# Gram products ahead of the merge, keys in four loads, one head per Gram matmul

## The reference, cut to what matters

```python
# r, k, v, w, a, b: [4 batches, 8 heads, 768 tokens, 40]
for t in range(S):
    y[:, :, t] = einsum('bhd,bhde->bhe', r_t, state)
    Sa = einsum('bhde,bhe->bhd', state, a_t)
    state = state * w_t[:, :, None, :] - einsum('bhd,bhe->bhde', Sa, b_t) \
            + einsum('bhd,bhe->bhde', v_t, k_t)
# then on y: x @ w_in, relu, a convolution of 3 taps over the tokens, a gate, @ w_out,
# and per batch an FFT over tokens and width, a normalization, and two more matmuls
```

## Time and profile before

| | us |
|---|---|
| median of 3 runs (1068.22 to 1072.94) | 1071.59 |
| the profiled execution's own time | 1070.56 |
| its span | 1068.7 |
| PE busy in it | 874.5 |
| DVE busy in it | 627.3 |
| ACT busy in it | 455.8 |
| POOL busy in it | 246.4 |

### The profile page before, as it was taken

One profiled execution on the slowest core, in us unless ns is written; L12 is line 12 of the kernel. 1 busy time (PEld: TensorE's weight loads), 2 busy tenths in 40 slices (PEclk: granted clock), 3 DMA queues, 4 the chain that ended last, 5 costly groups with the idle time before them and its releaser, 6 DMA issues.

```text
span 1068.7 us, 26585 instructions
## 1 busy us (share of the span) xinstructions
PE 874.5 (82%) x11476; PEld 829.9 (78%) x11476; DVE 627.3 (59%) x1109; ACT 455.8 (43%) x791; POOL 246.4 (23%) x236
## 2 busy tenths in 40 slices
PE   1658878878789699796686799887998779988798
PEld 1657777777778688795685799877998769987698
DVE  3684974965966957904596514765137652377522
ACT  2437356365365274273663313643136421264211
POOL 4326336245345353324232200000000000000000
PEclk9859989989979889889797899988999979998899
DMA  9501351451351351161331101001010010100001
GB/s 296 198 21 42 127 164 42 127 164 42 126 164 47 122 165 42 22 194 40 100 99 37 45 1 37 1 1 45 1 37 1 1 34 11 38 1 1 1 1 37
DMA packets 46245, 71.46 MB, mean 67 GB/s; under 512 B 27105, under 2 KB 37986, under 8 KB 42210
## 3 DMA queue, kind: packets, MB, share of 16 engines
q1 hardware_dynamic: 46130, 69.77, 20.4%
HBM read 61.89 MB, written 7.86 MB: 65 GB/s over the span
## 4 chain that ended last, share of the span: by engine, by line
PE 38%; DVE 11%; ACT 3%; issue 1%; DMA 0%; POOL 0%; SPq 0%; DVEq 0%; POOLq 0%; ACTq 0%
PE psum L1164 16%; PE psum L1172 15%; PE psum L1213 3%; PE psum L1232 2%; DVE gs L1035 2%; DVE cv L1081 1%; DVE cv L1079 1%; ACT cv L962 1%; PE psum L1155 1%; DVE stats L1122 1%; DVE tok L1050 1%; DVE gf L1089 1%; ACT hp L956 1%; DMA tok<-y_scratch 0%; DVE res L1117 0%
## 5 line engine op out<-in xcount | busy, mean ns | idle before, releaser
L1164 PE MATMUL psum<-xs,w 128*128 128x384 f32 x1152 | 216.9, 342 | 21.2 <-DVE xs L1071 12.2
L1172 PE MATMUL psum<-w,gs 128*128 128x320 f32 x1296 | 207.9, 316 | 18.6 <-DVE gs L1035 18.5
L1164 PEld LDWEIGHTS psum<-xs,w 128*128 128x128 f32 x1152 | 203.2, 191 | 23.6 <-DVE xs L1071 12.3
L1172 PEld LDWEIGHTS psum<-w,gs 128*128 128x128 f32 x1296 | 199.6, 193 | 22.4 <-DVE gs L1035 17.5
L1143 DVE SCALAR_TENSOR_TENSOR gs<-psum,gs 128x384 fp32r<-128x384 f32 x80 | 44.7, 558 | 151.6 <-ACT gs L1009 151.6
L1009 ACT ACTIVATE gs<-psum 128x384 fp32r<-128x384 f32 x80 | 39.3, 491 | 157.3 <-PE psum L1164 157.3
L472 DVE TENSOR_TENSOR inv<-inv,outer 128x31 f32<-128x31 f32 (+15 forms) x186 | 98.5, 529 | 6.4
L379 POOL TENSOR_TENSOR score<-score,mask 128x512 f32<-128x512 f32 x48 | 65.6, 1388 | 127.6 <-ACT score L594 127.5
L470 DVE TENSOR_TENSOR outer<-low,inv 128x31 f32<-128x31 f32 (+15 forms) x186 | 80.5, 433 | 4.5
L455 DVE TENSOR_TENSOR gram_k<-bank,mask 128x512 f32<-128x512 f32 x24 | 16.6, 692 | 110.8 <-PE bank L640 110.8
L900 POOL MEMSET xs<- 128x217 f32 x8 | 2.0, 278 | 285.4 <-ACT hp L956 285.4
(11 more groups left out here) (120 smaller groups left out, 1613.1 us busy)
## 6 DMA issues: line engine op xcount, KB each, us to landing
kb<-in_kb SPq DMA_DIRECT2D x6, 2048.0 KB, 8.5
rt<-in_rt SPq DMA_DIRECT2D x12, 1024.0 KB, 5.9
w_in<-in_w SPq DMA_DIRECT2D x6, 1040.5 KB, 9.9
at<-in_a SPq DMA_DIRECT2D x6, 1024.0 KB, 5.5
zt<-in_vt SPq DMA_DIRECT2D x12, 512.0 KB, 7.7
v_tok<-in_v SPq DMA_DIRECT2D x6, 640.0 KB, 7.7
y_scratch<-y_t SPq DMA_DIRECT2D x48, 80.0 KB
out<-res SPq DMA_DIRECT2D x24, 160.0 KB, 1.9
```

The lines of the kernel that those rows point to most:

```text
L1164: last = mm(ps[6 + half][:, 0:HALF], a[:, 128 * f:128 * f + 128], x[:, HALF * half:HALF * (half + 1)], start=(i == 0), stop=(i == len(ever ...
L1172: last = mm(ps[t][:, 0:DM], gs[:, f % 2, x, 128 * t:128 * t + 128], w[:, y, f, :], start=(f == 0 and i == 0), stop=(f == count - 1 and i = ...
```

## The change

`attention_jobs` gets a new order, `vector_order` goes, and `prep` is cut into `scan` (one for each b), `at`, `decays`, `eye` and `ends`. The copies `odd` and `blank` and the second half of the tile `at` go. A Gram matmul takes one head, with 64 rows of the array; the heads of one bank are those of eight pairs, the two row halves alternating with the two column halves. The minus-signed products are kept in two tiles (`gram_b`, `gram_m`), and `inv_1`, `merged` move to a tile of their own. The diagonal copies become a job `diag`, behind `mt`, and swap the heads of a pair for one chunk. `kb` is loaded in four pieces.

```diff
+    def grams(g, halves=range(2)):
+        return [("gram", g, kind, 2 * half + flip) for half in halves for kind in (0, 1) for flip in range(2)] if g < STEPS else []
...
+    def merge(g, beside):
+        order = each("mj", g, 0, 2) + beside + each("mt", g, 0, 2) + one("diag", g)
+        return order + [("pu", g, half, b) for b in batches for half in range(2)]
+
+    SUBS = (0, 10, 11, 17, 28, Q - 1)
+
+    order = each("scan", 0) + one("at", 0) + one("decays", 0) + each("keys", 0) + one("ends", 0)
+    order += interleave(grams(0), each("scan", 1)) + each("ta", 0) + one("eye", 0) + one("split", 0)
+    early = each("tb", 0, 1) + each("tb", 0, 0) + each("akv", 0) + one("at", 1) + one("decays", 1) + each("keys", 1)
+    order += interleave(early, subs(0, 0, 26)) + one("ends", 1) + interleave(grams(1), subs(0, 26, Q - 1))
+    order += one("unsplit", 0) + one("eye", 1) + merge(0, []) + one("split", 1) + subs(1, 0, SUBS[1])
     for g in range(STEPS):
         if g + 1 < STEPS:
-            order += interleave(grams(g + 1), state(g, 0, ("sat", "sa")))
-            beside = interleave(state(g, 0, ("st", "xn", "y", "xt")) + state(g, 1, ("sat", "sa", "st", "xn")),
-                                tokens(g + 1)[:-NB])
-            order += interleave(beside, chain(g + 1)[:-1]) + state(g, 1, ("y",)) + chain(g + 1)[-1:] + prep(g + 2)
-            order += merge(g + 1)[:2] + tokens(g + 1)[-NB:] + merge(g + 1)[2:] + spread(g + 1) + state(g, 1, ("xt",))
+            order += one("decays", g + 1) if g else []
+            first = interleave(each("sat", g, 0, 2) + each("sa", g, 0), each("ta", g + 1) + each("tb", g + 1, 1))
+            first += each("st", g, 0)
+            order += interleave(first, each("scan", g + 2) + subs(g + 1, SUBS[1], SUBS[2]))
+            second = each("xn", g, 0) + zipped(each("y", g, 0), each("tb", g + 1, 0)) + each("xt", g, 0, 2)
+            order += interleave(second, subs(g + 1, SUBS[2], SUBS[3])) + one("at", g + 2)
+            keys = each("keys", g + 2)
+            third = interleave(each("sat", g, 1, 2) + each("sa", g, 1), each("akv", g + 1)) + keys[0:2]
+            third += each("st", g, 1) + keys[2:4] + each("xn", g, 1)
+            order += interleave(third, subs(g + 1, SUBS[3], SUBS[4])) + one("ends", g + 2)
+            order += interleave(each("y", g, 1), subs(g + 1, SUBS[4], SUBS[5])) + one("unsplit", g + 1) + one("eye", g + 2)
+            last = grams(g + 2, (1,))
+            order += grams(g + 2, (0,)) + last[:2] + merge(g + 1, last[2:] + each("xt", g, 1, 2))
+            order += one("split", g + 2) + subs(g + 2, 0, SUBS[1])
...
@@ SyncE
-            if stage == "gram" and (c, b) == (0, NB - 1) and more:
+            if stage == "scan" and b == NB - 1 and more:
+                load_w(g + 1)
+            if stage == "ta" and b == NB - 1 and more:
                 load_a(g + 1)
             if stage == "akv" and b == NB - 1 and more:
-                load_w(g + 1)
                 load_v(g + 1)
-            if stage == "tb" and (c, b) == (1, NB - 1) and more:
-                load_kb(g + 1)
+            if stage == "tb" and c == 0 and more:
+                load_kb(g + 1, b)
...
@@ ScalarE
-                nc.scalar.mul(gram_b[0:2 * Q, heads, :], grams[0:2 * Q], -1.0)
-                nc.scalar.mul(gram_b[2 * Q:4 * Q, heads, 0:Q], grams[2 * Q:4 * Q, :, Q:C], -1.0).then_inc(drained[bank], 1)
+                nc.scalar.mul(gram_b[:, slots_b, :], grams[:, :, 0:Q], -1.0)
...
+                nc.scalar.mul(gram_m[:, g % 2, slots_b, :], grams[0:2 * Q, :, Q:C], -1.0).then_inc(drained[bank], 1)
...
@@ TensorE
-                for i, n in enumerate(pairs):
...
+                for i in range(NH):
+                    n = b // 2 * NH + i
+                    for q in range(1 if c == 0 else 2):
                         for cc in range(2):
+                            k = (b + cc) % 2
+                            r = slice(C * k, C * k + C)
+                            if c == 0:
+                                last = mm(out[C * cc:C * cc + C, i, :], kb[r, n, cc, 0, :],
+                                          at_quarters[r, n, :, cc, :], start=True, stop=True)
+                            else:
                                 p = Q * (2 * q + cc)
+                                last = mm(out[p:p + Q, i, 0:C - Q * q], kb[r, n, cc, 1, Q * q:Q * q + Q],
+                                          at_quarters[r, n, q:2, cc, :], start=True, stop=True)
```

More of the change, by code:

```diff
@@ L63, in attention_jobs, with each, one, subs @@
     batches = range(NB)
-    def prep(g):
-        return [("prep", g, 0, 0)] + [("keys", g, 0, b) for b in batches] if g < STEPS else []
-    def grams(g):
-        jobs = [("odd", g, 0, 0)] + [(stage, g, 0, b) for b in batches for stage in ("ta", "blank")]
-        return jobs + [("gram", g, kind, b) for kind in (1, 0) for b in batches]
-    def chain(g):
-        return [("split", g, 0, 0)] + [("sub", g, 0, i) for i in range(Q - 1)] + [("unsplit", g, 0, 0)]
-    def tokens(g):
-        jobs = [(stage, g, 0, b) for stage in ("akv",) for b in batches]
-        return jobs + [("tb", g, c, b) for c in range(2) for b in batches]
-    def merge(g):
-        return [("mj", g, 0, 0), ("mj", g, 0, 1), ("mt", g, 0, 0), ("mt", g, 0, 1)]
-    def spread(g):
-        return [("pu", g, half, b) for b in batches for half in range(2)]
-    def state(g, c, stages):
-        return [(stage, g, c, b) for stage in stages
-                for b in range(2 if stage in ("sat", "xt") else NB)]
+    def each(stage, g, c=0, n=NB):
+        return [(stage, g, c, b) for b in range(n)] if g < STEPS else []
+    def one(stage, g):
+        return [(stage, g, 0, 0)] if g < STEPS else []
+    def grams(g, halves=range(2)):
+        return [("gram", g, kind, 2 * half + flip) for half in halves for kind in (0, 1) for flip in range(2)] if g < STEPS else []
+    def subs(g, lo, hi):
+        return [("sub", g, 0, i) for i in range(lo, hi)] if g < STEPS else []
     def interleave(a, b):
@@ L115, in attention_jobs @@
-    return order
-def vector_order(order):
-    out, held = [], []
-    for job in order:
-        if job[0] == "y" and job[2] == 1 and job[1] + 1 < STEPS:
-            held.append(job)
-        else:
-            out.append(job)
-        if job[0] == "unsplit":
-            out += held
-            held = []
-    return out
-NOT_PSUM = ("prep", "table", "keys", "odd", "blank", "split", "sub", "unsplit")
+            order += one("decays", g + 1) if g else []
+            first = interleave(each("sat", g, 0, 2) + each("sa", g, 0), each("ta", g + 1) + each("tb", g + 1, 1))
@@ new lines, in attention_jobs @@
+            order += interleave(third, subs(g + 1, SUBS[3], SUBS[4])) + one("ends", g + 2)
[3 more added lines that the diff above has]
+            order += one("split", g + 2) + subs(g + 2, 0, SUBS[1])
+        else:
+            order += [(stage, g, 0, b) for stage in ("sat", "sa", "st") for b in range(2 if stage == "sat" else NB)]
+            rest = each("xn", g, 0) + each("y", g, 0) + each("xt", g, 0, 2)
+            rest += each("sat", g, 1, 2) + each("sa", g, 1) + each("st", g, 1)
+            order += interleave(rest, [("table", g, 0, i) for i in range(FIRST_PIECES)])
+            order += each("y", g, 1)
@@ L135, in first_tables @@
+    return order
+NOT_PSUM = ("scan", "at", "decays", "keys", "ends", "eye", "table", "split", "sub", "unsplit", "diag")
 def first_tables(nc, ctx, dram):
@@ L208, in attention @@
     s_a = sem("s_a")
-    s_kb = sem("s_kb")
+    s_kb = [sem(f"s_kb{i}") for i in range(NB)]
     s_rt = [sem(f"s_rt{c}") for c in range(2)]
@@ L302, in _ @@
         sp.dma_start(ident[:, :], dram["ident"]).then_inc(s_const, 16)
-        load_kb(0)
+        for b in range(NB):
+            load_kb(0, b)
         sp.dma_start(mask[:, :], dram["mask"]).then_inc(s_const, 16)
@@ L415, in _ @@
         dve.wait_ge(s_slots, 3)
-        for job in vector_order(order):
+        for job in order:
             stage, g, c, b = job
-            if stage == "prep":
+            if stage == "scan":
                 dve.wait_ge(s_w, 16 * (g + 1))
```

150 lines of the change are left out of this document (71 added, 79 removed).

## The result

The changed kernel takes 1114.97 us (median, 1106.96 to 1120.8), the kernel before 1072.26 us beside it on the same chip (1068.22 to 1073.4): a ratio of 1.04, interval 1.0328 to 1.0472. It is slower by 42.7 us, and the forecast of 1078 us and its range up to 1098 us both miss it. The profiled execution has a span of 1105.2 us against 1068.7 us: 36.5 us more. It was the shortest of the four, 8 us under their median, so differences of traces come out smaller here than differences of medians.

A forecast was written before the change was run, and what follows sets the result against it. A ring of waits, no engine full, bounds the kernel. Middle step: 77.6 - 18.7 + 9.5 + 1.0 + 7.4 = 76.8, taken as 77.7; start and turns add 6.1 to 1070.56, giving 1078 us; own range 1062 to 1098, overall 1034 to 1098.

The forecast's parts named there:

- the ring: Recurrence step: subs, `unsplit`, scans, `at` and keys, products, subs; opening it removes VectorE's 18.7 us wait, without net gain.
- (a): `at` and keys moved beside subs 11 to 27: GpSimd and VectorE alternate by instruction, costing 9.5 us a step.
- (e): Start, first and last turns, end: first T +22.7, first turn -4.6, last turn -12.3, end 0; whole +6.1 us.
- (b): After T (start of `inv_1`): VectorE's 18.7 us wait goes; waits of 1.0 before `split`, 7.4 before scans come.
- The bound of 11 us on the scans' wait: Upper bound on VectorE's wait for `decays`, predicted 7.4 us, if TensorE runs at 1.2 GHz around `mj`.
- (c): Gram products: kind 1 at 14.8 ns, kind 0 at 34 ns, together 8.2 us as today: nothing.
- row halves of one bank don't run together: Rival on the Gram products: done one at a time, 10.7 us more TensorE a step, 1110 us; chance 0.03.
- (d): Dropping `odd` and `blank` (1.9 + 2.5 us of ScalarE a step) gains nothing more; key loads and strides nearly free.
- The rivals: Other outcomes: TensorE setting the pace 0.24, half the added waits 0.11, keys late 0.07, row halves serial 0.03.
- TensorE sets the pace: Rival for the middle steps: VectorE's lock loss absorbed, a step about 67.5 us, whole 1036 us; chance 0.24.

The follow-up runs named there:

- after: The changed kernel itself, as measured and profiled against the kernel before: 1114.97 us, ratio 1.04.
- The run with the old order: New Gram products, four key loads and dropped copies, but jobs ordered as in the kernel before: 1084.37 us, ratio 1.0114 to the kernel before.
- kind 1 twice: The changed kernel with every kind 1 Gram product issued a second time into the same place: 1141.2 us, ratio 1.0646 to the kernel before.
- the two kernels with GpSimd's waits, early and late loads: Changed kernel with diagonal and decays copies early and GpSimd waiting on itself: 1070.93 us; the same with chunk 1's loads held until `mt` is drained: 1060.94 us.

## Why the prediction failed, point by point

**The reading of the ring** was right. So was the forecast that a middle step wins nothing by opening it: VectorE's 18.7 us went and came back.

**(a) The lock.** 9.5 us were put down. VectorE's busy time of a step rose by 62.8 - 56.6 = 6.2 us, the subs' from 31.6 to 35.7 to 36.5, not to 38 to 42. So the sum was too high by 3. In the start it was met: the subs of step 0 take 31.9 us instead of 21.2, the 10.7 more that (e) put down. The form was wrong too: turns for each instruction, as in the earlier trace rows, where a single block came. The Trainium skill, "SBUF — State Buffer", "Who interferes with whom", has the loser of the shared port blocked for the whole instruction of the other. Here it was blocked for six instructions; with a wait between them, for one each. The page's rule holds for the scores, and is too mild for a run of GpSimd instructions without a wait.

**(b) The waits of VectorE: the step that failed.** 1.0 + 7.4 = 8.4 us were predicted. In the three middle turns it was 5.43 + 11.70, 7.42 + 10.49 and 7.83 + 9.08: 17.3 us in the mean, 8.9 more, and the step came out 8.2 us longer than predicted. (The terms shown for `split` add up to T + 6.9, not T + 7.6, so even the 1.0 was 0.3 by its own sum.) The two waits had been found, with their right releasers. Both were priced with the running time of `mj`, kind 1, `mt` and `pu`, as if TensorE could be fed at that pace. In the turn at 240.14 `pu` was to start at T + 13.7 and started at T + 20.8. Of the 7.1 us, 1.1 are the late `mj` behind the first stop, 3.02 + 0.82 + 0.41 = 4.25 the stops in it and behind it, and 1.4 the diagonal copies: 3.49 us of wait instead of 2.1, since ScalarE drains the last `mt` bank first. `pu` took 9.22 us instead of 7.5, partly at 1.2 GHz: 1.7 more. The bound of 11 us on the scans' wait, for a TensorE at 1.2 GHz, held in two turns of three; `split` had been given no bound at all, and there the wait was five to eight times the 1.0 us. A third wait was denied: VectorE was never to wait between the scans and the next T, and it waits 2.64, 3.52 and 3.70 us for `xn` of chunk 1. With it the sum of a middle turn closes. Before, on the mean: 56.5 busy + 18.9 wait for kind 0 + 2.4 in small gaps = 77.8. After: 62.8 + 17.3 + 3.3 + 2.4 = 85.8, measured 85.9.

**(c) The products** take what they were said to take, 15.5 and 30 ns, and "nothing" was still wrong, in a way that no row of a single product shows. A step has 1669 matmuls instead of 1456, and where they are short TensorE needs 3.5 to 4.8 us for each 127 of them with quiet queues. Such stops are in the kernel before too, and no row of them was read for the prediction. The longest stands in the turn from 295.38 us:

```profile
354.66 0.69 PE L695 MATMUL bank<-pu,xi 80*64 80x64 f32 x7 [4.87 <-issue]
```

Counted by the packet that lands ahead of them, these stops sum to 3.4, 3.2 and 5.8 us in the three middle turns of before and to 3.3, 6.0 and 5.5 us in those of after. So the change added less than 1 us a turn of them. What it changed is their place: between T and `pu` before has none, and after has 3.1, 6.0 and 5.3 us, in the stretch that VectorE waits for. (The 1.8 us without a releaser inside the Gram products of one step of before are of another kind: they end 2.5 and 4.8 us behind a packet.) The run with the old order shows a second cost that was missed, the bank that waits for two pieces of keys. That row halves of one bank don't run together was rejected, rightly.

**(d)** Nothing was seen against it.

**(e) The start** was good to 3 us (81.6 for 84.8), the first turn to 1.3 (-3.3 for -4.6), the end to 1.6. The last turn was wrong by 10: 75.3 for 65.3. It was summed from TensorE's busy time, 56.5 us, plus waits of 5 us. TensorE is busy for 61.3 us of it, at a clock of 0.86, stands still for 6.3 us with the releaser "issue", and waits the same 3.49 us for the copies ahead of `pu`. The account closes: the middle turns have 24.1 - 0.3 = 23.8 us more than predicted, and 10.0 + 1.3 - 3.1 - 1.6 = 6.6, together 30.4, which is 36.5 - 6.1.

**The rivals.** None of them had this mechanism. "TensorE sets the pace" had the right engine for the waits in (b), but counted it with no time but its busy time, and so on the other side.

**What stays open.** How much of the 9.2 us of `pu` is due to the stops by way of the clock wasn't isolated: in the middle turns `pu` took 8.2 to 10.0 us in every variant of the new order, those with short stops too, and 7.2 to 7.4 us in the old order, where TensorE runs without a long stop from `mj` to `pu`. No run took the stops away, so their share of the late `pu` (4.25 of 7.1 us in one turn) is read from a trace. Whether the late packet is asked for late or held up in its queue behind the loads' packets, the trace doesn't tell.

## What to carry to other kernels

Where an engine runs many short instructions, price them by count as well as by duration: look for idle time with the releaser "issue" at equal distances, see whether a packet of the instruction queue lands just ahead of its end, and take the time from stop to stop, not the time of the instructions. When a wait is opened by reordering, list what every in-order queue now holds between the old releaser and the new waiter; the places of two copies of 2 us each were worth 39 us here. And keep bulk loads out of a stretch in which an engine lives on the supply of its instructions.

## What the runs showed of the hardware

- TensorE stops after 126 or 127 pairs of weight load and matmul, if these are short: 31 + 96, 32 + 94, 34 + 16 + 76. Doubled products shift the stop to another job at the same count (225 and 227). The stops end 1.2 to 1.6 us behind the landing of a packet of 16,384 bytes on the instruction queue: 15 of 15 in after, 25 of 25 with kind 1 twice.
- A block of 127 short pairs takes 3.5 to 4.8 us from stop to stop with quiet queues (after and the two kernels with GpSimd's waits, early and late loads) and 5.8 to 7.6 us beside the chunk loads, once only 4.2; the DMA engines' share up to the landing of the packet is then 0.97 or more. The pairs alone run in 2.3 to 3.2 us. Where 128 pairs take 3.50 or 3.62 us at 1.2 GHz, no stop shows behind them; behind 94 in 2.40 us there it is 0.82 us. By the Trainium skill, "SBUF — State Buffer", "Who interferes with whom", a transfer never contends with a compute engine. That is said of SBUF ports; by way of the instructions it does here: a stop of 3.92 us beside the loads is 2.00 us without them, and the kernel goes from 1070.93 to 1060.94 us.
- GpSimd keeps VectorE out over instructions that follow each other without a wait: one sub of 0.42 us lasted 9.59 us beside six of them. When each is followed by a wait on its own semaphore, six subs of 0.94 to 2.96 us take its place.
